# The attention stage of a fused attention and expert kernel: TensorE's order inside a token tile, the bank of the row transposes, and the queue that loads the gate weights

## The reference

```python
def _attn_ref(q, k, v):                      # (2, 8, 768, 64)
    gamma = 1.0 - 2.0 ** (-5.0 - np.arange(H))
    for t in range(S):
        state = gamma * state + k[:, :, t] (outer) v[:, :, t]
        y[:, :, t] = scale * q[:, :, t] @ state
# x = y as (1536 tokens, 512)
logits = x @ w_gate                          # (512, 8), argmax picks the expert
# per expert, capacity 384: relu(x @ w1[e]) @ w2[e], times the gate weight
# then h = x @ w_in; g = P(h) / Q(h); out = g @ w_out
```

## Time and profile before

| | |
|---|---|
| median of 3 runs | 536.76 us (536.65 to 537.22) |
| profiled execution | 536.65 us, of which its span is 534.8 us |
| PE busy | 525.8 us, 98% of the span |
| DVE, ACT, POOL busy | 423.5, 329.6, 76.4 us |
| chain that ended last | PE 96%, DMA 1%, DVE 1%, SP's queue 1% |
| granted TensorE clock | 1.00, the 2.4 GHz level |

### The profile page before, as it was taken

One profiled execution on the slowest core, in us unless ns is written; L12 is line 12 of the kernel. 1 busy time (PEld: TensorE's weight loads), 2 busy tenths in 40 slices (PEclk: granted clock), 3 DMA queues, 4 the chain that ended last, 5 costly groups with the idle time before them and its releaser, 6 DMA issues.

```text
span 534.8 us, 8739 instructions
## 1 busy us (share of the span) xinstructions
PE 525.8 (98%) x3209; PEld 439.0 (82%) x3209; DVE 423.5 (79%) x759; ACT 329.6 (62%) x508; POOL 76.4 (14%) x74
## 2 busy tenths in 40 slices
PE   6999999999999999999999999999999999999997
PEld 4888888888888888888788888888888888888885
DVE  2578788785856759577989999997888888787886
ACT  2464546584655747457969867658566566655652
POOL 3343342260101101003010010004000000200000
PEclk9999999999999999999999999999999999999999
DMA  9999959959968384903060000003000000200002
GB/s 194 232 247 254 275 199 392 396 147 389 380 237 303 149 332 144 398 29 99 23 217 1 1 21 20 1 1 113 7 21 20 1 0 1 80 1 0 0 1 79
DMA packets 65087, 72.26 MB, mean 135 GB/s; under 512 B 41234, under 2 KB 41746, under 8 KB 65044
## 3 DMA queue, kind: packets, MB, share of 16 engines
q1 hardware_dynamic: 58596, 57.96, 34.5%
q0 software_dynamic: 3136, 9.46, 5.2%
q10 hardware_dynamic: 3312, 4.28, 2.3%
HBM read 59.09 MB, written 12.60 MB: 134 GB/s over the span
## 4 chain that ended last, share of the span: by engine, by line
PE 96%; DMA 1%; DVE 1%; SPq 1%; issue 0%; ACT 0%
PE up_low L949 7%; PE up_low L950 7%; PE up_low L951 7%; PE bank L949 6%; PE bank L950 6%; PE bank L951 6%; PE up_high L955 6%; PE up_low L955 5%; PE yrows L949 4%; PE yrows L950 4%; PE up_high L951 4%; PE up_high L949 4%; PE up_high L950 4%; PE yrows L951 4%; PE up_high L956 3%; PE up_low L956 3%
## 5 line engine op out<-in xcount | busy, mean ns | idle before, releaser
L876 DVE TENSOR_TENSOR T<-raw,T 128x1024 fp32r<-128x1024 f32 x60 | 71.5, 1219 | 33.8 <-ACT T L870 33.8
L870 ACT ACTIVATE T<-raw 128x1024 fp32r<-128x1024 f32 x60 | 60.5, 1070 | 32.2 <-PE bank L951 31.8
L949 PE MATMUL up_low<-x2H,T 128*128 128x512 f32 x176 | 69.3, 394 | 0.0
L951 PE MATMUL up_low<-x2H,T 128*128 128x512 f32 x176 | 68.5, 389 | 0.0
L950 PE MATMUL up_low<-x2L,T 128*128 128x512 f32 x176 | 68.5, 389 | 0.0
L1529 ACT ACTIVATE sq<-up_low 128x512 f32<-128x512 f32 x44 | 26.2, 596 | 64.4 <-PE up_low L951 64.1
L1550 DVE SCALAR_TENSOR_TENSOR wa<-sq,coef,wa 128x512 f32<-128x512 f32 x48 | 35.9, 748 | 28.7 <-ACT wa L1531 28.7
L949 PE MATMUL bank<-T,hL 128*128 128x512 f32 x128 | 50.6, 395 | 0.0
L951 PE MATMUL bank<-T,hH 128*128 128x512 f32 x128 | 49.9, 390 | 0.0
L950 PE MATMUL bank<-T,hH 128*128 128x512 f32 x128 | 49.8, 389 | 0.0
L1543 ACT ACTIVATE rc<-wa,cst 128x512 f32<-128x512 f32 x48 | 34.8, 725 | 20.6 <-DVE wa L1550 15.9
(11 more groups left out here) (205 smaller groups left out, 1228.7 us busy)
## 6 DMA issues: line engine op xcount, KB each, us to landing
raw<-in_moe_w_dram SPq DMA_DIRECT2D x14, 2048.0 KB, 10.9
raw<-in_moe_w_dram SPq DMA_DIRECT2D x8, 512.0 KB, 5.1
w_out_raw<-in_moe_w_out_dram SPq DMA_DIRECT2D x4, 1024.0 KB, 17.1
ybuf<-ysb ACTq DMA_DIRECT2D x15, 256.0 KB
qin<-in_q_dram SPq DMA_DIRECT2D x12, 256.0 KB, 5.3
kin<-in_k_dram SPq DMA_DIRECT2D x12, 256.0 KB, 5.7
vin<-in_v_dram SPq DMA_DIRECT2D x12, 256.0 KB, 5.6
xbuf<-xt SPq DMA_DIRECT2D x12, 256.0 KB, 4.2
```

Source lines behind the costliest of these rows:

```text
L870: e.activation(W[w][:, 0, cols], raws[par][:, w, cols], ACT.Copy).then_inc(r.wH[w], 1)
L876: e.tensor_tensor(W[w][:, 1, cols], raws[par][:, w, cols], W[w][:, 0, cols].bitcast(F32), ALU.subtract).then_inc(r.wL[w], 1)
L949: nc.tensor.matmul(out_, aL, bH, start=start, stop=False)
L951: return nc.tensor.matmul(out_, aH, bH, start=False, stop=stop)
```

## The change

Four edits. R goes to bank 0, shared with Q' in place of K, and moves behind QS. S of a tile moves from the end of the tile before to a place behind A. ACT copies qT directly behind kT and the state after both. The last load of constants and the four gate loads go from ACT's queue to SP's, between the loads of tile 1 and those of tile 2.

```diff
 def pe_transpose_qk(t):
             e.wait_ge(s_lk[t % LB], t // LB * 16 + 16)
             wait(e, s_ek, t)
-            if t >= 3:
-                e.wait_ge(s_x, rows_done(t - 3))
             for p in range(HP):
                 last = e.transpose(bank[1][...], qkv[t % LB][1][...], ident)
             last.then_inc(s_tk, 1)
             ...
             wait(e, s_qs, t)
             wait(e, s_eq, t)
+            if t >= 3:
+                e.wait_ge(s_x, rows_done(t - 3))
 def rows_bank(t):
-            return bank[1] if t + 2 < NT else bank[4 + t - (NT - 2)]
+            return bank[0] if t + 2 < NT else bank[4 + t - (NT - 2)]
 def pe_rows(t):
-            e.wait_ge(s_ek, min(t + 3, NT))
+            e.wait_ge(s_eq, min(t + 3, NT))
-        def act_load_gate():
...
-        def act_evac_k(t):
...
-        def act_evac_q(t):
...
+        def act_evac_qk(t):
             e = nc.scalar
             wait(e, s_y, t - 1)
+            for bk, dst, tr, done in ((1, kT, s_tk, s_ek), (0, qT, s_tq, s_eq)):
+                e.wait_ge(tr, t + 1)
+                e.activation(dst[t % 2][...], bank[bk][:, :], ACT.Copy).then_inc(done, 1)
 def pe_first_tile():
             pe_state(0)
             pe_scores(1)
             pe_values(0)
-            pe_state(1)
 def pe_tile(t):
             pe_logits_apart(t - 1)
-            pe_rows(t - 1)
-            pe_logits_sum(t - 1)
+            if t % C < C - 1:
+                pe_state(t)
+                pe_logits_sum(t - 1)
             if t % C:
                 pe_query_state(t)
+            if t % C == C - 1:
+                pe_logits_sum(t - 1)
+            pe_rows(t - 1)
             pe_scores(t + 1)
             if t >= 2:
                 pe_index(t - 2)
             pe_positions(t - 1)
             pe_values(t)
-            if (t + 1) % C < C - 1:
-                pe_state(t + 1)
 def act_tile(t):
             if t + 1 < NT:
-                act_evac_k(t + 1)
+                act_evac_qk(t + 1)
             if t % C < C - 1:
                 act_state(t)
-            if t + 1 < NT:
-                act_evac_q(t + 1)
 SP:
                 load_v(t)
+            e.dma_start(cst[:, lay["kdecay"][1]:CW], consts[:, lay["kdecay"][1]:CW]).then_inc(s_cst, 16)
+            e.wait_ge(s_zm, 2)
+            gate_rows = w_gate.rearrange("(u c r d) e -> c r d u e", u=2, c=2, r=2)
+            for c in range(2):
+                for r in range(2):
+                    e.dma_start(wg[...], gate_rows[c, r, :, :, :]).then_inc(s_wg, 16)
             load_q(2)
             load_k(2)
             load_v(2)
 ACT:
             e.preload_act_table_set("natural_log_exp_and_others")
-            e.dma_start(cst[:, lay["kdecay"][1]:CW], consts[:, lay["kdecay"][1]:CW]).then_inc(s_cst, 16)
-            act_load_gate()
-            act_evac_k(0)
-            act_evac_q(0)
+            act_evac_qk(0)
```

More of the change, by code:

```diff
@@ L437, in pe_x_late @@
                     last.then_inc(s_x0, 1)
-        def act_load_gate():
[L442 to L447, removed]
-        def act_evac_k(t):
+        def act_evac_qk(t):
             e = nc.scalar
             wait(e, s_y, t - 1)
-            e.wait_ge(s_tk, t + 1)
-            e.activation(kT[t % 2][:, :, :].rearrange("p a b -> p (a b)"), bank[1][:, :], ACT.Copy).then_inc(s_ek, 1)
-        def act_evac_q(t):
[L456 to L459, removed]
+            for bk, dst, tr, done in ((1, kT, s_tk, s_ek), (0, qT, s_tq, s_eq)):
+                e.wait_ge(tr, t + 1)
+                e.activation(dst[t % 2][:, :, :].rearrange("p a b -> p (a b)"), bank[bk][:, :], ACT.Copy).then_inc(done, 1)
         def act_evac_xT(t):
@@ L1750, in _ @@
                 load_v(t)
+            e.dma_start(cst[:, lay["kdecay"][1]:CW], consts[:, lay["kdecay"][1]:CW]).then_inc(s_cst, 16)
[3 more added lines that the diff above has]
+                for r in range(2):
+                    e.dma_start(wg[c * D:(c + 1) * D, 2 * r:2 * r + 2, 0:E], gate_rows[c, r, :, :, :]).then_inc(s_wg, 16)
             load_q(2)
```

## The result

| | before | after |
|---|---|---|
| median | 536.76 us (536.65 to 537.22) | 540.11 us (538.93 to 542.42, 5 runs) |
| profiled execution, its span | 536.65, 534.8 us | 542.69, 540.9 us |
| start of V in tile 10 | 68.83 | 75.09 |

The change makes the kernel slower: the ratio is 1.0058, with a 95% interval of 1.0031 to 1.0086. The forecast of 537.4 was 2.7 us too low, and its range ended at 538.9. The new kernel also scatters more. Its eight executions run from 538.53 to 542.69. Those with a mean granted clock of 0.999 or 1.0 took 538.5 to 539.9, the one at 0.997 took 540.1, and the three at 0.993 and 0.994 took 541.4 to 542.7. The profile shown is the slowest of the eight.

The account below looks back on a forecast made before the run. PE was taken to bound the kernel (busy 98% of the span). Start -0.1, six tiles +0.84, tiles 5 and 6 +0.04 and 0, tile 7 -0.34, load stall +0.3: +0.74, from 536.65 to 537.4 us; range 536.1 to 538.9.

Parts of the forecast that it names:

- The start: Opening, K of tile 2: its load lands at 14.9, V of tile 1 starts at 19.5 against 19.59, -0.1.
- The slow rival: Start: gate loads hold up SP in full, k of tile 2 lands at 16.5, total 538.7; chance 0.27.
- The second rule: Start: issuing on several engines saves little, so k lands at 13.8 and the start gives 1.1 more.
- K to V: Tile 1, from K of tile 2 to V of tile 1: 4.63, where it was 4.11.
- A tile, after: Full tile on PE in the new order: nine joints sum to 5.66, 0.14 more than 5.52.
- The rule weighed in the prediction: PE's tiles: 0.10 for each change of shape, minus the wait of 0.12, gives +0.08 a tile.
- The wait for kT: R's wait in each tile for the copy of kT in bank 1: it goes, worth 0.12 a tile.
- Tiles 5, 6 and 7: Tiles without S, without QS, and with the stall: 5.10, 5.06, and 5.66 in place of 6.00 (0.34 saved).
- the cover that I counted on: Tile 6: R between L and Sc gives 2.09 between logits and V, so tile 7 has no stall.
- The loads that PE then meets: Tile 8: k of tile 9 lands at 53.6, PE at 53.65, a stall of 0.3 on top.
- the 0.5 of slip: SP's list: later stores delay the k load of tile 9 by 0.5, from 53.1 to 53.6.
- The sum: Whole kernel: +0.44 on PE plus 0.3 of load stall, +0.74, from 536.65 to 537.4.

Follow-up runs that it names:

- `after_again`: The changed kernel run once more without any edit, in the third batch: 540.07 us (539.51 to 541.12, 5 runs).
- `sp_queue`: The kernel before with only the constants load and the four gate loads moved to SP: 538.51 us, ratio 1.0023.
- `act_order`: The kernel before with only ACT's copy order changed to kT, qT, state: 536.24 us, ratio 0.9983.
- `act_order2`: The kernel before with only ACT's copy order changed to kT, qT, state, repeated in the third batch: 537.13 us, ratio 0.9985.
- `act_queue`: The changed kernel with the constants load and the four gate loads back on ACT's queue: 537.49 us, ratio 1.0004.
- `a_first`: The kernel before with A between K and Q' in tiles with S, ACT's new order, DVE's weights piece before its choice: 538.02 us, ratio 0.999.
- `gates_act`: The changed kernel with the four gate loads back on ACT, the constants load still on SP: 537.82 us, ratio 0.9998.
- `short_filler`: The changed kernel with twelve small zero products (2.94 us) on PE behind V of tile 0: 543.21 us (6 runs).
- `r_late`: `act_queue` with S put back behind V, so that of PE's order only R is moved: 542.68 us, ratio 1.0086.

## Why the prediction was wrong, step by step

**The start: this step failed.** It put the landing of k at 14.9, a little below the middle of 13.8 and 16.5, because SP waits for its queue anyway and would swallow part of the issue time. SP swallowed hardly any. The five DMAs and the q load take from 7.08 to 11.58; the wait that shrank is that of the q load (0.60 in place of about 1.26), and k left 3.14 later, more than the 2.70 that was the step's upper bound. For it counted the four gate loads alone: the load of constants, 1.14 of SP's time, had no price. K started at 16.81 in the one profile and at 15.63 in the other, 1.91 and 0.73 behind the forecast. The slow rival had the mechanism and, for the first of the two, the landing (16.5), at a chance of 0.27; its 538.7 lies among the executions at full clock (538.5 to 539.9). The second rule, by which k would have landed at 13.8, fails: k landed at 15.6 and 16.7, since the issue of the four loads of 4 KB took 2.67 us, about as long as each of them took to land (2.1 to 2.8).

**The clock: no step and no rival had it.** K to V was to take 4.63. At full clock it took 4.73 (`after_again`); in the profile of after, at 1.2 GHz for most of it, it took 7.70. The clock cost 2.97 us there, and with the 1.91, and 0.1 for the tile's joints, it makes the 5.0 by which V of tile 1 missed the 19.5. I read the clock of before as 1.00 throughout and never asked what an idle PE would do to it. The Trainium skill, TensorE: Matmul & The Clock Gate, HAM oscillation, describes a loop in which TensorE waits for a DMA in every pass, so that its clock falls and the next pass starts slow. The trace of after agrees, and with a single wait: 0.50 behind 2.93 us of idle time. Behind 1.84 the clock stayed at 1.00. The rule belonged to the slow rival, as its second price. Not every execution pays: at 0.993 to 0.994 three of eight did in the first set, and in `after_again` none of the five was below 0.996. Nor is it the changed kernel alone: of the 73 executions of the kernel before that ran beside the batches, five had a mean clock of 0.993 or 0.994, at 539.3 to 540.6. So the low clock goes with the three slowest of the first eight, and it isn't needed for the median of `after_again`. That the idle time lowers it is shown by one profile and argued from the runs with a filler.

**A tile, after: right in kind, 0.12 too small.** Seven of nine terms came within 0.01 (A to S 0.36, L to QS 0.32, QS to R 0.60). Two were mis-sized: S to L takes 0.61, for which I had taken S to K (0.56), and R to Sc 0.59, for which I had taken Q' to A (0.53) although the high end was 0.63. A full tile takes 0.26 more, not 0.14, and six of them 1.56 in place of 0.84. The rule weighed in the prediction, 0.10 for each change of shape, gave 0.08 and is further off. The wait for kT went as said, with A to S at 0.36.

**Tiles 5, 6 and 7.** 5.06 and 5.08 against 5.10 and 5.06. Tile 7 had no stall in the profile of after, and took 5.78 (a full tile). But in `after_again` it took 6.60, with L waiting 0.75. The tok write again started just behind POOL's decay (0.10 behind) and took 1.02, as before. DVE was late there because of the step before: `hot_all` took 0.64 in place of 0.23 and ended at 48.05, 0.03 behind POOL's scaling of q, which had waited 1.57 for its load:

```profile
46.98 1.04 POOL L629 TENSOR_TENSOR qs<-qin,cst 128x512 f32<-128x512 f32 x1 [1.57 <-DMA qin<-in_q_dram]
...
47.41 0.64 DVE L506 TENSOR_SCALAR hot_all<-rankv,rmax 128x8 bf16<-128x8 f32 x1
```

In the profile of after the two stand the other way round, 0.10 apart, and tok takes 0.23:

```profile
53.13 0.23 DVE L542 SCALAR_TENSOR_TENSOR tok<-hot_all,row_no,inside 128x24 f16<-128x24 bf16 x1
...
53.23 1.04 POOL L629 TENSOR_TENSOR vs<-vin,cst 128x512 f32<-128x512 f32 x1 [1.95 <-PE yrows L349]
```

So the cover that I counted on mostly works, but it is thin. All four profiles in which R and S stand where they stood (before, `sp_queue`, `act_order`, `act_order2`) have this stall in tile 7. Of the seven with the changed order one has it, where a late load took 0.4 of the cover. The Trainium skill, SBUF — State Buffer, SBUF: two separate sides, says that DVE and GpSimd share one pair of ports as an exclusive lock, and that the one which starts second is blocked. The profile of `after_again` agrees: tok ends at 50.62 and POOL at 50.60. The other way round nothing is seen here: in the profile of after POOL starts second and takes its usual 1.04.

**The loads that PE then meets: not met.** In the profile of after, PE was 5 us later than forecast, and the load with it: k of tile 9 is issued at 51.60, lands 6.5 later, at 58.1, and K uses it at 58.8 without a wait. `act_queue`, with its start as early as before, uses that k at 53.24 without a wait, where the step had it land at 53.6. It was issued 0.23 later than before (45.94 against 45.71), less than the 0.5 of slip, and took 6.8 in place of 7.4. The limit itself is real: `a_first` met it with 0.32, at 52.96, near the 53.1 that the step gave without a slip.

```profile
53.24 0.66 PE L263 MATMUL up_low<-cst,kin 128*128 128x128 f32 x4
```

**The sum.** From V of tile 1 to V of tile 10 the forecast had +0.84 over before (six joints 0.84, +0.04, -0.34, loads 0.30); measured +1.34. These 0.50 and the 5.01 of the start are the 5.5 by which V of tile 10 (75.09) missed the forecast's 69.57. By `after_again`, whose profile is near its median, V of tile 10 is 3.34 behind the profile of before, which is not of its batch: 0.77 at tile 1, 2.57 behind it, which are the joints of seven full tiles (1.82), a tok collision that cost 0.34 more than before's, a wait of 0.29 for the k of tile 3, and 0.12 of small differences. Set against the forecast (69.57) it is 2.60 behind, and only 0.86 of this is the start: 0.94 is tile 7 (6.60 in place of 5.66) and 0.72 the joints of six tiles. In its own batch the kernel is 2.20 above before.

**What the parts are worth.** In the first batch: order and bank with the loads left on ACT, 1.0004 (0.9993 to 1.0015), no change that can be told; ACT's order alone, 0.9983, and 0.9985 in the third. So the order on PE, the bank and R's place cost about what ACT's order brings, and the gate loads on SP make the result: in the third batch the changed kernel is 2.20 us above before, and `gates_act` takes back 2.25.

## What to carry to other kernels

Where DMAs are moved to a queue that also feeds the critical engine, count their issue time in full against the next load on that queue, and find out first whether that load has slack; four loads of 4 KB cost 2.67 us of it here. Where a forecast has the matrix engine idle for a few microseconds, give it a rival in which the clock falls behind the idle time and the matrix work of some microseconds takes up to twice as long (here it cost 3 us in one execution and nothing in another). Price a joint between two groups only by the same pair of groups, and take the upper bound where that pair has not been seen.

## What I had not expected of the hardware

Behind an idle time of 1.75 us at the end of the attention the clock stood at 0.51 for 10 us in `short_filler` and at 0.50 for over 3 us in `r_late`, while behind 1.84 us at the start it stayed at 1.00: what idle time costs is not read from its length alone. A write of 128x8 numbers by DVE took up to 1.10 us in place of 0.23 where POOL worked beside it, and that held up PE. The landing of the same load varied from 4.0 to 5.1 us after the same issue. And a stall of a microsecond, as of K on the rows' copy or of L on lgT, is there in one execution of a kernel and not in the next, so that one profile shows one of several ways through the same program.
